# A convolution and two MLPs on one core: turning tokens with 32 by 32 blocks on VectorE and DMAs instead of transposes on TensorE

## The reference

```python
# x: (2, 4096, 192), weight_gen: (2, 4096, 8, 7)
w = softmax(weight_gen, axis=-1)                   # 7 taps for each token and head
out[b, s, h, :] = sum_k w[b, s, h, k] * x[b, s - 6 + k, h * 24:(h + 1) * 24]   # zeros ahead of s = 0
y = out.reshape(8192, 192)
h = np.maximum(y @ w_in1, 0.0)                     # (192, 2048)
y = h * h @ w_out1                                 # (2048, 192)
h = y @ w_in2
y = (h * np.clip(h + 3.0, 0.0, 6.0) / 6.0) @ w_out2
```

## Time and profile before

| | |
|---|---|
| median of 3 runs | 1181.51 us (1180.98 to 1181.69) |
| the profiled execution | 1181.42 us, of which its span is 1179.6 us |
| TensorE busy | 1167.7 us (99%) |
| VectorE busy | 898.2 us (76%) |
| ScalarE busy | 686.5 us (58%) |
| DMA queue of SP | 12828 packets, 31.19 MB, 8.2% of 16 engines |
| granted TensorE clock | 0.998 of full speed |

### The profile page before, as it was taken

The page is one execution under the profiler, slowest core; times in us unless marked ns, Lnnn a source line. Parts: engine busy times, 40 slices in busy tenths (PEclk is TensorE's granted clock), DMA queues, the critical chain, the costliest instruction groups (busy, mean ns, idle before and its releaser), DMA issues.

```text
span 1179.6 us, 26311 instructions
## 1 busy us (share of the span) xinstructions
PE 1167.7 (99%) x10800; PEld 1155.2 (98%) x10800; DVE 898.2 (76%) x998; ACT 686.5 (58%) x802; POOL 3.7 (0%) x11
## 2 busy tenths in 40 slices
PE   7999999999999999999999999999999999999998
PEld 7999999999999999999999999999999999999997
DVE  8888787787868778687786877868688786876554
ACT  6886655656555565655556455565555556555554
POOL 1000000000000000000000000000000000000000
PEclk9999999999999999999999999999999999999999
DMA  7211001000000101000010000100001010000000
GB/s 210 80 62 53 1 19 34 17 33 0 17 33 17 33 0 51 0 17 33 0 51 0 17 33 15 36 0 17 33 17 33 0 46 5 13 0 2 14 1 28
DMA packets 12860, 31.65 MB, mean 27 GB/s; under 512 B 1184, under 2 KB 7710, under 8 KB 12828
## 3 DMA queue, kind: packets, MB, share of 16 engines
q1 hardware_dynamic: 12828, 31.19, 8.2%
HBM read 24.89 MB, written 6.29 MB: 26 GB/s over the span
## 4 chain that ended last, share of the span: by engine, by line
PE 97%; ACT 1%; DMA 1%; DVE 1%; issue 1%; SPq 0%; DVEq 0%; ACTq 0%
PE h_ps L794 45%; PE y_ps L805 30%; PE y_ps L814 20%; PE y_ps L899 1%; DMA stage<-in_moe_w_out_dram 0%; PE y_ps L906 0%; DMA outs<-in_x_dram 0%; DVE acc L529 0%; ACT hid L368 0%; PE y_ps L912 0%; ACT hid L363 0%; DVE wout L582 0%; ACT hid_hi L376 0%; SPq L272 0%; DVE prod L551 0%
## 5 line engine op out<-in xcount | busy, mean ns | idle before, releaser
L794 PE MATMUL h_ps<-xt,win 64*128 64x512 f32 (+1 forms) x4860 | 1022.7, 379 | 0.7 <-DVE wout L582 0.7
L794 PEld LDWEIGHTS h_ps<-xt,win 64*128 64x128 f32 x4860 | 806.4, 185 | 1.8 <-DVE wout L582 1.1
L805 PE MATMUL y_ps<-hid_hi,wout 64*128 64x512 f32 (+1 forms) x2160 | 566.1, 381 | 0.3 <-DVE win L582 0.3
L609 DVE TENSOR_TENSOR hid_lo<-hid,hid_hi 128x1024 fp32r<-128x1024 f32 (+1 forms) x270 | 313.0, 1159 | 172.6 <-ACT hid_hi L379 166.4
L379 ACT ACTIVATE hid_hi<-hid 128x1024 fp32r<-128x1024 f32 (+1 forms) x244 | 256.3, 1050 | 310.8 <-DVE hid L600 143.8
L805 PEld LDWEIGHTS y_ps<-hid_hi,wout 64*128 64x128 f32 x2160 | 372.7, 185 | 7.7 <-DVE win L582 0.5
L814 PE MATMUL y_ps<-hid_lo,wout 64*128 64x512 f32 (+1 forms) x1080 | 327.6, 383 | 0.0
L814 PE MATMUL y_ps<-hid_hi,wout 64*128 64x512 f32 (+1 forms) x1080 | 323.0, 378 | 0.0
L805 PE MATMUL y_ps<-hid_lo,wout 64*128 64x512 f32 (+1 forms) x1080 | 322.8, 378 | 0.0
L805 PEld LDWEIGHTS y_ps<-hid_lo,wout 64*128 64x128 f32 x1080 | 194.9, 184 | 0.6 <-DVE hid_lo L609 0.4
L814 PEld LDWEIGHTS y_ps<-hid_hi,wout 64*128 64x128 f32 x1080 | 195.2, 185 | 0.3
(11 more groups left out here) (80 smaller groups left out, 356.1 us busy)
## 6 DMA issues: line engine op xcount, KB each, us to landing
xwin<-in_x_dram SPq DMA_DIRECT2D x14, 960.0 KB
out_dram<-outs SPq DMA_DIRECT2D x16, 384.0 KB, 2.5
stage<-in_moe_w_out_dram SPq DMA_DIRECT2D x8, 384.0 KB, 6.1
stage<-in_moe_w_in_dram SPq DMA_DIRECT2D x4, 512.0 KB, 5.2
stage<-in_moe_w_in_dram SPq DMA_DIRECT2D x8, 256.0 KB, 5.3
wraw<-in_weight_gen_dram SPq DMA_DIRECT2D x16, 112.0 KB, 2.3
xwin<-in_x_dram SPq DMA_DIRECT2D x1, 768.0 KB
outs<-in_x_dram SPq DMA_DIRECT2D x2, 216.0 KB, 3.5
```

Of the source, the lines that this page charges most:

```text
L609: dve.tensor_tensor(lo, hid[:, slot, :, 0:width], hi.bitcast(fp32), ALU.subtract).then_inc(lo_done, 1)
L794: return pe.matmul(h_ps[:, s % 2, t, 0:tokens.stop - tokens.start], win[layer][r, wn, cols], src[r, xn, tokens], start=bool(rows) and n in ...
L805: return pe.matmul(ps[:, 0, tokens], wout[layer][r, tile, w_cols], src, start=bool(rows) and s == 0 and n == 0, stop=not rows and s == STE ...
```

## The change

In the loop TensorE transposes no more. For chunks 3 to 15 VectorE turns every 32 by 32 block of `acc` in place of `turn_att` (`turn_tokens`, in step 10), and SP moves the blocks to their partitions with 24 DMAs inside SBUF (`move_blocks`); the staging buffers of the weights, no longer used then, hold both. The split reads SBUF instead of PSUM. So that step 10 is free, all taps are done one step earlier (steps 3 to 9). For chunks 0 to 14 the sums are copied out with the factor 1/6, VectorE turns their 32 by 32 blocks in step 12 (`turn_out` on VectorE), and 32 DMAs write them to the output rows in pieces of 128 bytes (`store_turned`). `copy_out` goes. `copy_o` now waits for the stores of the chunk before. Chunk 15 goes out as before. The order of tokens in a chunk's columns is another for chunks from 3 on (`VECTOR`), which the DMAs' addresses take in. The three first iterations of SP's loop are written out.

```diff
+    STORES = 16 * J * (P // Q + 2 * (REST // Q))
...
+        xs_main, xs_rest = stage[:, 0, 0:N], stage[REST:P, 1, 0:N]
+        blocks = stage[:, 2, 0:J * D]
...
+            def move_blocks(c):
+
+                sp.wait_ge(x1_lo, 2 * c + 4)
+                sp.wait_ge(prep_done, prep_value(c, "turn_main"))
+                for f in range(P // Q):
+                    for b in range(PBLOCKS):
+                        sp.dma_start(xs_main[f * Q:(f + 1) * Q, b * P:(b + 1) * P],
+                                     blocks[b * Q:(b + 1) * Q, f * P:(f + 1) * P]).then_inc(x_main_moved, 16)
+                sp.wait_ge(prep_done, prep_value(c, "turn_rest"))
+                for f in range(REST // Q):
+                    for b in range(PBLOCKS):
+                        sp.dma_start(xs_rest[f * Q:(f + 1) * Q, b * P:(b + 1) * P],
+                                     blocks[b * Q:(b + 1) * Q, N + f * P:N + (f + 1) * P]).then_inc(x_rest_moved, 16)
+
+            def store_turned(c):
...
+                sp.wait_ge(out_turned, 2 * c + 1)
+                for f in range(P // Q):
+                    for row in range(J):
+                        sp.dma_start(target(f, row), columns(main[f * Q:(f + 1) * Q], row)).then_inc(out_stored, 16)
+                sp.wait_ge(out_turned, 2 * c + 2)
+                for half in range(2):
+                    for f in range(REST // Q):
+                        p0 = half * REST + f * Q
+                        for n in range(J):
...
+                            sp.dma_start(target(P // Q + f, row)[:, b0:b0 + 2], src).then_inc(out_stored, 16)
...
-            with sp.Fori(2, CHUNKS - 2) as i:
-                store_chunk(i - 2)
-                load_chunk(i + 2)
...
+            def iteration(i):
+                sp.wait_ge(exp_done, i + 2)
+                load_gates(i + 2)
+                move_blocks(i + 1)
+                load_window(i + 2)
+                store_turned(i - 2)
...
+            def split_moved_hi(c, dst, free):
+
+                act.wait_ge(mm1_done, free)
+                act.wait_ge(x_main_moved, 16 * PBLOCKS * (P // Q) * (c - (VECTOR - 1)))
+                act.activation(dst[:, 0, :], xs_main, ACT.Copy).then_inc(x1_hi, 1)
+                act.wait_ge(x_rest_moved, 16 * PBLOCKS * (REST // Q) * (c - (VECTOR - 1)))
+                act.activation(dst[REST:P, 3, :], xs_rest, ACT.Copy).then_inc(x1_hi, 1)
...
                 act.wait_ge(mm2_done, steps)
                 if not isinstance(c, int) or c >= 1:
-                    act.wait_ge(out_turned, c)
+                    act.wait_ge(out_turned, 2 * c)
+                    act.wait_ge(out_stored, STORES * c)
...
+            def turn_tokens(c):
...
+                done(dve.transpose(blocks[:, 0:N].rearrange("p (f j q) -> p f j q", j=J, q=Q), turned_acc[:, 0:P // Q]))
+                done(dve.transpose(blocks[:, N:J * D].rearrange("p (f j q) -> p f j q", j=J, q=Q), turned_acc[:, P // Q:D // Q]))
+
+            def turn_out(c):
+                dve.wait_ge(o_copied, 2 * c + 2)
+                dve.wait_ge(o_added, c + 1)
+                dve.transpose(out_main, o_main).then_inc(out_turned, 1)
+                dve.transpose(out_rest, o_rest).then_inc(out_turned, 1)
...
-                    if 4 <= s < 4 + TAPS and prep:
-                        taps(i + 1, [s - 4])
+                    if 3 <= s < 3 + TAPS and prep:
+                        taps(i + 1, [s - 3])
+                    if s == 3 + TAPS and prep:
+                        turn_tokens(i + 1)
+                    if s == 12:
+                        turn_out(i - 2)
...
                     second_body(g0 + s, inn, out_of(s - LAG - 1), out_of(s - LAG))
-                    if s == 5:
-                        turn_out(i - 2)
-                    if s == 13 and prep:
-                        turn_att(i + 1, y1_ps)
```

More of the change, by code:

```diff
@@ new lines, in store_turned, with target, columns @@
+            def store_turned(c):
+                main = out_main.rearrange("p (n q) -> p n q", q=Q)
+                rest = out_rest.rearrange("p (n q) -> p n q", q=Q)
+                row_first = isinstance(c, int) and c < VECTOR
+                def target(f, row):
+                    return out_blocks[f][:, :, bass.ds(c * J + row, 1), :].rearrange("t b r q -> t b (r q)")
+                def columns(blocks_of, row):
+                    if row_first:
+                        return blocks_of[:, row * PBLOCKS:(row + 1) * PBLOCKS, :]
+                    return blocks_of.rearrange("p (b r) q -> p r b q", r=J)[:, row]
+                sp.wait_ge(out_turned, 2 * c + 1)
[7 more added lines that the diff above has]
+                        for n in range(J):
+                            row, b0 = (half * JHALF + n // 2, n % 2 * 2) if row_first else (n, half * 2)
+                            src = rest[p0:p0 + Q, 2 * n:2 * n + 2, :] if row_first else columns(rest[p0:p0 + Q], n)
+                            sp.dma_start(target(P // Q + f, row)[:, b0:b0 + 2], src).then_inc(out_stored, 16)
@@ L311, in _ @@
                 load_piece(n)
-            load_chunk(2)
+            sp.wait_ge(exp_done, 2)
+            load_gates(2)
+            load_window(2)
             for n in range(PIECES + STAGES, 2 * PIECES):
                 load_piece(n)
-            load_chunk(3)
-            with sp.Fori(2, CHUNKS - 2) as i:
-                store_chunk(i - 2)
-                load_chunk(i + 2)
+            sp.wait_ge(exp_done, 3)
+            load_gates(3)
+            load_window(3)
+            def iteration(i):
[4 more added lines that the diff above has]
+                store_turned(i - 2)
+            for i in range(2, VECTOR + 2):
+                iteration(i)
+            with sp.Fori(VECTOR + 2, CHUNKS - 2) as i:
+                iteration(i)
+            move_blocks(CHUNKS - 1)
             for c in range(CHUNKS - 4, CHUNKS - 1):
[L320 to L323, removed]
+                store_turned(c)
+            store_last(CHUNKS - 1)
+            sp.wait_ge(out_stored, STORES * (CHUNKS - 1) + 16)
         @block.gpsimd
@@ L443, in iteration @@
                     if s == 14 and prep:
-                        split_x1_hi(i + 1, xt[0], y1_ps)
+                        if isinstance(i, int) and i + 1 < VECTOR:
+                            split_x1_hi(i + 1, xt[0], y1_ps)
+                        else:
+                            split_moved_hi(i + 1, xt[0], g0 + STEPS)
                     relu(g0 + s, s // STEPS, s % 2)
@@ L534, in taps @@
                         if not isinstance(c, int) or c >= 1:
-                            dve.wait_ge(att_turned, c + 2 if half is None else half + 1)
+                            dve.wait_ge(att_turned, half + 1 if half is not None else c + 2 if isinstance(c, int) else VECTOR + 2)
                         if not isinstance(c, int) or c >= 1:
@@ L625, in add_o @@
                 dve.wait_ge(o_copied, 2 * c + 2 - final)
-                dve.tensor_tensor(o_rest[0:REST, :], ps[0:REST, 1, 0:HALF], o_cross[:, 0:HALF], ALU.add)
-                dve.tensor_tensor(o_rest[REST:P, :], ps[0:REST, 1, HALF:N], o_cross[:, HALF:N], ALU.add).then_inc(o_added, 1)
+                for half, rows in enumerate((slice(0, REST), slice(REST, P))):
+                    if final:
+                        js = slice(half * JHALF, (half + 1) * JHALF)
+                        ins = dve.tensor_tensor(o_rest[rows, :].rearrange("p (j b i) -> p j b i", j=JHALF, i=Q),
+                                                by_row(ps[0:REST, 1, :])[:, js], row_major(o_cross)[:, js], ALU.add)
+                    else:
+                        cols = slice(half * HALF, (half + 1) * HALF)
+                        ins = dve.scalar_tensor_tensor(out=o_rest[rows, :], in0=ps[0:REST, 1, cols], scalar=1.0 / 6.0,
+                                                       in1=o_cross[:, cols], op0=ALU.mult, op1=ALU.add)
+                ins.then_inc(o_added, 1)
             def iteration(i, prep, last):
@@ L900, in turn_att, with turn_last_out @@
                 ins.then_inc(att_turned, 1)
-            def turn_out(c, final=0):
+            def turn_last_out():
                 for j in range(J):
@@ L913, in turn_out, with iteration @@
                                            ident[r, r], tile_position=(r.start, 0))
-                ins.then_inc(out_turned, 1)
-            def iteration(i, prep, last):
+                ins.then_inc(last_turned, 1)
+            def iteration(i):
                 g0 = first_step(i) if isinstance(i, int) else pe.snap(i * (2 * STEPS) + STEPS)
```

91 lines of the change are left out of this document (50 added, 41 removed).

## The result

| | before | after |
|---|---|---|
| median | 1181.56 us (6 runs, 1180.88 to 1182.42) | 1185.85 us (6 runs, 1185.30 to 1187.45) |
| ratio | | 1.0038, 95% interval 1.0025 to 1.0051 |
| the profiled execution | 1181.42, span 1179.6 | 1185.75, span 1183.8 |

What follows compares the result with a forecast made beforehand. TensorE, busy for 99% of the span and 97% of the chain, was taken as the bound. From 1181.42 us, 7.15 for turn_att and 6.45 for turn_out came off, the rest costing nothing: 1168 us, range 1165 to 1191.

Steps and rivals of the forecast that it cites:

- The savings: TensorE's loop: 13 turn_att at 0.55 us and 15 turn_out at 0.43 us go, together 13.6 us.
- VectorE: Steps 10 and 12: a pair of turns takes 1.1 us (bounds 0.8 and 4.4), covered by idle time, cost nothing.
- dear turns: Rival, VectorE: turns at 4.4 us a pair start the moves 2 us later; 1177 us with issues at 0.47; chance 0.05.
- The moves: SP from step 10: 24 issues at 0.42 us, all landed at 407.9, 2.5 us ahead of need; cost nothing.
- the loaded queue: SP's issue price with queues full of weights, 1.08 us, taken as far bound; the time would be 1341 us.
- The slack: Moves, issued from 395.3 and due landed by 410.4: 12.6 us for 24 issues, 0.525 us each, with 2.5 us for landing.
- late moves: Rival: issues over 0.525 us hold ScalarE at step 14's split, the relu behind it; 1191 us at 0.6; chance 0.13.
- The stores: 32 stores behind the moves, 68 ns a packet, done by 427 at the latest, before copy_o needs them; cost nothing.
- slow small stores: Rival: 128-byte packets to HBM take 136 ns, so copy_o holds ScalarE 11 us beyond its slack; 1322 us; chance 0.07.
- A part of the gain only: Rival, TensorE's loop: small waits or a slower pace (0.04 us a step is 8 us); 1176 to 1182 us; chance 0.07.

Runs made afterwards that it cites:

- through_dram: Changed kernel with the 24 moves replaced by one write of the turned blocks to DRAM and 6 reads: 1169.82 us, 0.9900 of the kernel before.
- four_more_moves: Changed kernel with 4 more moves of the same size into an unread staging buffer, ahead of the rest: 1246.60 us, 1.0553 of the kernel before.

## Why the prediction was wrong

**The savings** were nearly right. With the wait taken away the kernel runs at 1169.5 where 1168 was forecast, 11.7 us less than before on its chip instead of 13.6. An iteration takes 70.93 us and not 70.8, because its steps run at 4.433 us and not at the 4.424 that the steps without transposes took before.

**VectorE** was right: the turns took 0.70 and 0.40 us where 0.68 and 0.42 were taken; *dear turns* fell with that. The Trainium skill, VectorE: DVE Perf Modes, The three transpose paths, gives 311 ns for 128 x 128 in bf16; an estimate from it, four times that, is 1.24 us for the main turn. This trace shows 0.70 for fp32. The moves began at 396.91. Forecast were 395.3 in an iteration whose copy_o stood at 357.03; here it stands at 358.91, so that is 397.2.

**The moves: here a step failed.** "I take 0.42" for one issue of a move; it was 0.63, and with it the "Cost: nothing" of the moves became 1.4 us in each of 13 iterations. The row nearest in kind, four DMAs back to back at 0.45, was undercut rather than taken. It was also of another form: a load from DRAM. No row showed a DMA from SBUF to SBUF, and I called the loaded queue the far bound and leaned to the low end, with no reason that a row gives. The slack itself was reckoned too small, since a landing takes 1.8 us and not 2.5: with the end of the wait 1.4 us earlier, (411.8 - 1.8 - 396.9) / 23 = 0.57 us an issue was the limit. So the place, the relu queued behind the copy of step 14, and the form of the loss were foreseen as *late moves*, at 13% and priced at 1191 for 0.6 us; with the landing that was measured, 0.63 gives 13 x 23 x 0.06 = 18 us over 1168, and so 1186.

**The stores** cost nothing, as forecast, but not for the reason given. A packet took 11.5 ns and not 68, and *slow small stores* fell. The 68 ns were not a price "for up to 768 bytes" either: the 1447 packets of the earlier trace rows hold 1.72 MB, which is 1.2 KB each. What set the end of the stores were again the issues, at (429.29 - 412.96) / 32 = 0.51 us instead of 0.42, behind moves that ended late. They landed at 430.4, after the 427 that was called the latest, and 0.5 us ahead of copy_o. The Trainium skill, DMA: Bandwidth & Descriptors, Specifications, says that below 512 B a transfer does not reach line rate, by a read-modify-write. This trace does not speak against it: an engine moved 0.24 MB / (14.2% x 16 x 11 us) = 9.6 GB/s while busy, and 17.4 in the earlier trace rows. But a packet of 128 bytes took a sixth of the time of those packets, not twice that time.

**A part of the gain only** fell as well: apart from the one wait, no step of the loop is over 4.44 us. The pace that it named did show once the wait was gone, but at 0.01 us a step, about 2 us in all, and not 8.

**What the chances missed.** A cover of 12.6 us over 24 identical steps turns on a unit price, and an error of 0.1 us in it is 31 us of the time. With the unit price between 0.33 and 1.08 in the rows, and the limit in the lower part of that, 13% for the wrong side of it was far too little.

## What to carry to other kernels

Count DMA instructions, not bytes, when a burst of them feeds a wait: on SP's queue each took 0.44 to 0.63 us from one issue to the next, by its form, and a quarter of the bytes changed nothing. Here a second queue, or a detour through DRAM with 7 DMAs, beat 24 small moves. Where work waits for a transfer, put what TensorE needs next ahead of that wait in the same engine's queue; moving the copies of the rest behind one relu, and VectorE's part behind one gate, turned +0.4% into -1.0%. And when a forecast hangs on a unit price times a count, bound it by operations of the same form, and say how much of the price range lies beyond the limit.

## What the runs showed of the hardware that was not expected

The issue of a DMA on SP depends on its form. The rows of single lines (min/median/max ns, first and last start) for a move inside SBUF and a store with an address from a register in the kernel after, and for a read from DRAM with fixed addresses in through_dram:

```profile
L326 SPq DMA_DIRECT2D stage<-stage x208: 513/591/1279, 179.8 to 1055.1; - x104
```

```profile
L351 SPq DMA_DIRECT2D out_dram<-outs x240: 315/316/1932, 196.3 to 1166.5; - x120
```

```profile
L332 SPq DMA_DIRECT2D stage<-scratch x52: 315/432/434, 182.8 to 1035.3; - x52
```

Between two issues come 0.04 us more. Of the 240 stores of L351, 144 take their address from a register, which costs 0.07 us of register work ahead of each issue; so a store is about as dear with it as without: 16 take 7.90 us in the iteration shown, and the 16 with fixed addresses from 196.3 us on, at 0.43 us each, take 7.84. Why the form matters was not tried.

TensorE's clock: the idle times of 1.0 to 1.7 us, one in each iteration of the changed kernel, left the granted clock at 1.0 in every us of the loop. Idle times of 3.4 to 4.8 us in four_more_moves halved it in every iteration, for 6.8 us in the one shown and for half as long in six others. A transfer that is late enough is paid once by the wait and again by the clock.
